# Two sums of squares by accumulating transfers, and another queue for y

## The reference

```python
# q, k, v, a_re, a_im: [4, 8, 768, 48]
mag = np.sqrt(a_re * a_re + a_im * a_im)
scale = np.minimum(mag, 0.999) / (mag + 1e-06)
a_re_n, a_im_n = a_re * scale, a_im * scale
for t in range(S):                       # complex decay of a 48 x 48 state per head
    new_re = ar * S_re - ai * S_im
    new_im = ar * S_im + ai * S_re
    S_re, S_im = new_re + k[t] (x) v[t], new_im
    y[:, :, t] = np.einsum('bhd,bhde->bhe', q[:, :, t], S_re)
# x = y as [3072, 384]
h = x @ w_in                             # 384 -> 2048
x = softplus(h) @ w_out                  # 2048 -> 384
out = ((x @ w1) * (x @ w2)) @ w3 @ w_out2
```

## Time and profile before

| | us |
|---|---|
| median of 3 runs | 1011.33 (1008.62 to 1012.21) |
| time of the profiled execution | 1010.65 |
| its span, first to last instruction | 1008.9 |
| PE busy | 912.0 (90%) |
| DVE busy | 607.4 (60%) |
| ACT busy | 426.8 (42%) |
| POOL busy | 70.4 (7%) |

### The profile page before, as it was taken

The page is one execution under the profiler, slowest core; times in us unless marked ns, Lnnn a source line. Parts: engine busy times, 40 slices in busy tenths (PEclk is TensorE's granted clock), DMA queues, the critical chain, the costliest instruction groups (busy, mean ns, idle before and its releaser), DMA issues.

```text
span 1008.9 us, 14507 instructions
## 1 busy us (share of the span) xinstructions
PE 912.0 (90%) x5442; PEld 828.5 (82%) x5442; DVE 607.4 (60%) x966; ACT 426.8 (42%) x618; POOL 70.4 (7%) x56
## 2 busy tenths in 40 slices
PE   0964839999999999999989999987999999999998
PEld 0533739988999888989889999987888888888887
DVE  5977978989989989989899723445121212121211
ACT  3152254673764664853854654667011111212011
POOL 0000000000000000000000000000222222222221
PEclk9985569999999999999999999999999999999999
DMA  9676074381470570560650630232101010101000
GB/s 338 227 201 176 20 205 110 106 196 55 137 207 13 152 192 10 169 176 13 196 145 12 174 78 12 72 124 79 32 1 63 1 63 0 62 0 63 1 32 32
DMA packets 98663, 99.52 MB, mean 99 GB/s; under 512 B 6944, under 2 KB 91936, under 8 KB 98592
## 3 DMA queue, kind: packets, MB, share of 16 engines
q1 hardware_dynamic: 98592, 98.59, 34.1%
HBM read 63.96 MB, written 29.88 MB: 93 GB/s over the span
## 4 chain that ended last, share of the span: by engine, by line
PE 47%; DVE 28%; DVEq 9%; ACT 8%; issue 4%; DMA 3%; ACTq 1%; SPq 0%
PE ps_p L1281 5%; PE ps_p L1282 5%; PE ps_p L1283 5%; DVE sp L1165 4%; DVEq L921 3%; PE ps L1469 3%; PE ps L1467 3%; PE ps L1468 3%; DVE g_l L1172 2%; DVE am L1119 2%; PE ps L1281 2%; PE ps L1283 2%; PE ps L1282 2%; PE ps_ay L1317 2%; DVE an L953 2%
## 5 line engine op out<-in xcount | busy, mean ns | idle before, releaser
L1281 PE MATMUL ps<-g_h,wo_h 128*128 128x384 f32 x384 | 133.5, 348 | 7.1 <-DVE g_l L1172 7.1
L629 POOL TENSOR_TENSOR abl<-ab,abh 128x512 fp32r<-128x512 f32 x48 | 69.5, 1447 | 931.7 <-DVE abh L1263 931.7
L1281 PE MATMUL ps_p<-x1h,win_h 128*128 128x384 f32 x336 | 117.3, 349 | 15.7 <-DVE sp L1165 15.3
L1283 PE MATMUL ps<-g_h,wo_l 128*128 128x384 f32 x384 | 129.4, 337 | 0.0
L1282 PE MATMUL ps<-g_l,wo_h 128*128 128x384 f32 x384 | 129.1, 336 | 0.0
L1283 PE MATMUL ps_p<-x1h,win_l 128*128 128x384 f32 x336 | 113.1, 337 | 0.0
L1282 PE MATMUL ps_p<-x1l,win_h 128*128 128x384 f32 x336 | 113.0, 336 | 0.0
L745 ACT ACTIVATE g_h<-sp 128x768 fp32r<-128x768 f32 (+1 forms) x71 | 55.5, 781 | 98.2 <-DVE sp L1165 98.2
L1317 PE MATMUL ps_ay<-stq,stk 96*128 96x128 f32 x384 | 57.5, 298 | 34.7 <-DMA vt<-in_v 13.3
L1254 DVE TENSOR_TENSOR ab<-ps_ay,bc 128x512 f32<-128x512 f32 x24 | 16.6, 693 | 117.0 <-ACT bc L892 117.0
L1317 PEld LDWEIGHTS ps_ay<-stq,stk 96*128 96x128 f32 x384 | 54.9, 211 | 35.9 <-issue 23.4
(11 more groups left out here) (147 smaller groups left out, 2053.4 us busy)
## 6 DMA issues: line engine op xcount, KB each, us to landing
qk_scr<-tt SPq DMA_DIRECT2D x16, 576.0 KB, 4.5
stq<-qk_scr SPq DMA_DIRECT2D x48, 192.0 KB, 4.8
qk_scr<-pp SPq DMA_DIRECT2D x16, 576.0 KB, 4.1
stk<-qk_scr SPq DMA_DIRECT2D x48, 192.0 KB, 4.6
an<-in_a_re SPq DMA_DIRECT2D x8, 576.0 KB, 4.1
an<-in_a_im SPq DMA_DIRECT2D x8, 576.0 KB, 5.2
qk<-in_q SPq DMA_DIRECT2D x8, 576.0 KB, 7.5
qk<-in_k SPq DMA_DIRECT2D x8, 576.0 KB, 8.7
```

The lines of the kernel that those rows point to most:

```text
L629: tensor_tensor(abl[:, m % AR, :], ab[:, m % 2, :], abh[:, m % AR, :].bitcast(F32), ALU.subtract).then_inc(ab_lo, 1)
L1281: mm(o, wh, xh, start=start, stop=False)
L1283: return mm(o, wl, xh, start=False, stop=stop)
```

## The change

Both sums of squares leave VectorE. GpSimd, once the squares are there, begins a transfer that reads the second half of `te` and adds it onto the first half, and ScalarE waits for 16 on the semaphore where it waited for 1. `prep_m2_` and `prep_p2_` become empty. `store_y` moves from SyncE to GpSimd, with the waits that stood before it. GpSimd's order is that in which the work falls due: in tile m's attention, the sum for p of tile m + 1 after block 3 and the sum for a of tile m + 2 after block 4. Nothing else is moved.

```diff
--- before.py
+++ after.py
@@ -409,13 +409,6 @@
                     eng.dma_start(stk[D * i:D * i + D, :, cs], qk_scr[2 + i].rearrange("(h d) t -> d h t", d=D)[:, :, cs])\
                         .then_inc(k_rd[c], 16)
 
-            def store_y(m, i):
-                c, hq = i // 2, i % 2
-                wait(y_ev, NG * m + i + 1)
-                for u, row, rows, pairs, p0, gs_ in Y_MOVES[hq]:
-                    eng.dma_start(x1raw[p0:p0 + rows, gs_, CT * c:CT * c + CT], ys[64 * u + row:64 * u + row + rows, i % 2, pairs, :])\
-                        .then_inc(y_wr[i], 16)
-
             def load_x1(n, m):
 
                 for c0, rows, p0, g in PLACES:
@@ -467,10 +460,6 @@
             wait(w34_ev, NM2)
             eng.dma_start(w34_scr.rearrange("c p n -> p c n"), w34s[:, :, :]).then_inc(w34_wr, 16)
             load_piece(7)
-
-            wait(raw_lo, 5)
-            for i in range(NG):
-                store_y(0, i)
             wait(prep_p, 4)
             load_a(2)
             store_q(1)
@@ -486,29 +475,17 @@
 
                 if not first:
                     store_x2(n - 1)
-                if att:
-
-                    if first:
-                        wait(x1_lo, 2)
-                    else:
-                        x2_landed(n - 1)
-                    for i in range(NG - 2):
-                        store_y(n + 1, i)
                 if prep:
                     wait(prep_p, 2 * n + 6)
                     if nxt:
                         load_a(n + 3)
                     store_q(n + 2)
-                if att:
-                    store_y(n + 1, NG - 2)
                 if prep:
 
                     wait(yz_mm, NG * n + NG + 4)
                     for c in range(2):
                         stack_q(n + 2, c)
                         load_v(n + 2, c)
-                if att:
-                    store_y(n + 1, NG - 1)
                 if prep:
                     store_k(n + 2)
                     for c in range(2):
@@ -629,6 +606,45 @@
                 tensor_tensor(abl[:, m % AR, :], ab[:, m % 2, :], abh[:, m % AR, :].bitcast(F32),
                               ALU.subtract).then_inc(ab_lo, 1)
 
+            def store_y(m, i):
+                c, hq = i // 2, i % 2
+                eng.wait_ge(y_ev, NG * m + i + 1)
+                for u, row, rows, pairs, p0, gs_ in Y_MOVES[hq]:
+                    eng.dma_start(x1raw[p0:p0 + rows, gs_, CT * c:CT * c + CT], ys[64 * u + row:64 * u + row + rows, i % 2, pairs, :])\
+                        .then_inc(y_wr[i], 16)
+
+
+            def sum_squares(m):
+                eng.wait_ge(prep_sq, m + 1)
+                eng.dma_start(te[:, 0, :], te[:, 1, :], accum_op=ALU.add).then_inc(prep_m2, 16)
+
+            def sum_psquares(m):
+                eng.wait_ge(prep_psq, m + 1)
+                eng.dma_start(te[:, 0, :], te[:, 1, :], accum_op=ALU.add).then_inc(prep_p2, 16)
+
+            sum_squares(0)
+            sum_psquares(0)
+            sum_squares(1)
+
+            eng.wait_ge(raw_lo, 5)
+            for i in range(NG):
+                store_y(0, i)
+            sum_psquares(1)
+            sum_squares(2)
+            for m in range(1, NT):
+
+                if m == 1:
+                    eng.wait_ge(x1_lo, 2)
+                else:
+                    for mo in range(G):
+                        eng.wait_ge(x2_wr[mo], 16 * m)
+                for i in range(NG):
+                    store_y(m, i)
+                    if m < NT - 1 and i == 3:
+                        sum_psquares(m + 1)
+                    if m < NT - 2 and i == 4:
+                        sum_squares(m + 2)
+
             with eng.Fori(0, NT2) as t:
                 for m in range(NM2):
                     ab_low(t, m)
@@ -659,7 +675,7 @@
                 last.then_inc(prep_sq, 1)
 
             def prep_log(m):
-                eng.wait_ge(prep_m2, m + 1)
+                eng.wait_ge(prep_m2, 16 * m + 16)
                 act(te[:, 1, :], te[:, 0, :], ACT.Ln)
 
             def prep_root(m):
@@ -688,7 +704,7 @@
                     prep_psquare(m, i)
 
             def prep_inverse(m):
-                eng.wait_ge(prep_p2, m + 1)
+                eng.wait_ge(prep_p2, 16 * m + 16)
                 act(te[:, 1, :], te[:, 0, :], ACT.Ln)
                 eng.drain()
                 act(stats[:, 5 * m + 2:5 * m + 5].unsqueeze(2), by_g(te[:, 0, :])[:, :, T - 1:T], ACT.Copy).then_inc(end_ev, 1)
@@ -924,9 +940,7 @@
                 eng.drain()
 
             def prep_m2_(m):
-                eng.wait_ge(prep_sq, m + 1)
-                ve.tensor_tensor(te[:, 0, :], te[:, 0, :], te[:, 1, :], ALU.add).then_inc(prep_m2, 1)
-                eng.drain()
+                pass
 
             def prep_newton(m):
 
@@ -1013,9 +1027,7 @@
                 ve.tensor_tensor(tt[:, :, :], qk[:, 0:1, :].to_broadcast([P, 2, GT]), pp[:, :, :], ALU.mult).then_inc(prep_q, 1)
 
             def prep_p2_(m):
-                eng.wait_ge(prep_psq, m + 1)
-                ve.tensor_tensor(te[:, 0, :], te[:, 0, :], te[:, 1, :], ALU.add).then_inc(prep_p2, 1)
-                eng.drain()
+                pass
 
             def prep_inv_newton(m):
 
```

## The result

The change makes the kernel slower: 1095.2 us, median of 4 runs (1093.3 to 1098.4), against 1011.8 of the kernel before; ratio 1.083, 95% interval 1.081 to 1.085. The profiled execution has a span of 1096.6 us, 87.7 more than before; it is the slowest of the four (1098.4), so its losses add up to some 4 us more than the medians'.

The account below looks back on a forecast made before the run. It put 47% of the span on TensorE and 28% on VectorE. Terms 31.2 + 22.0 + 19.4 + 5 = 77.6 us on 1010.65 gave 1088 us, own range 1065 to 1105, 8 in 10 between 1036 and 1140.

Parts of the forecast that it names:

- Two waits of ScalarE, passed on: Before both Ln ScalarE waits for the transfer; TensorE then idles 4 to 5 us twice in a slot.
- |p|^2, 5.2 us late: Slots 0 to 5: the |p|^2 transfer takes 7.0 us, making its Ln 5.2 us late, six times: 31.2 us.
- |a|^2, 4.4 us late: Slots 0 to 4: the |a|^2 transfer takes 6.0 us, making its Ln 4.4 us late, five times: 22.0 us.
- Start, 19.4: Before the slots, four late sums (7.6, 4.2, 4.1, 3.5 us) count in full; |a|^2 of tile 2 counts nothing: 19.4 us.
- Clock, 5: TensorE's lower clock after new stops costs 1 us in each of five slots: 5 us.
- y at nothing: y's 192 issues moving from SyncE to GpSimd count 0, with +4 us a slot as upper end.
- A: Rival: the addition lands like a plain copy, in 3.6 us; 24.6 us in all, 1035 us; chance 0.20.
- The estimate of 4.7 us: Transfer time for 1.18 MB by the skill's rule and straight line; the sum would be about 41 us, 1051 us.
- B: Rival: the transfer is slow, 10 us like the k load in a full queue; 125 us, 1136 us; chance 0.15.
- C: Rival: GpSimd's issues at 2 us each hold up the |a|^2 sum by 3.8 us; 19 us on top, 1107; chance 0.10.
- D: Rival: transfers land within 1.84 us (|p|^2) and 1.57 us (|a|^2); VectorE's 14.9 us come back, 996 us; chance 0.05.

Follow-up runs that it names:

- sums_alone: Kernel after, with y's moves back on SyncE, so only the two sums become GpSimd's accumulating transfers; 1094.2 us, ratio 1.082.
- hidden_p2: Kernel after, with |a|^2 summed on VectorE and the next step's softplus ahead of the |p|^2 Ln, other preparation later; 1049.7 us, ratio 1.037.
- m2_alone: Kernel after, with the sum of |p|^2 back on VectorE, so only |a|^2 is summed by a transfer; 1052.0 us, ratio 1.040.
- quiet_p2_alone: Kernel after, with |a|^2 summed on VectorE and SyncE's next a loads and q-product store held until the |p|^2 sum lands; 1057.6 us.
- y_alone: Kernel before, with only y's moves put on GpSimd and both sums still VectorE additions; 1013.7 us, ratio 1.0016.
- quiet: Kernel after, but in the slots SyncE begins the next a's loads and q-product store only once the |p|^2 sum has landed; 1095.7 us.
- sliver: Kernel after, but each transfer adds only 16 of 1152 columns (8 KB) and VectorE the other 1136 beside it; 1047.6 us, ratio 1.036.
- q_on_pool: Kernel before, with the product of q and the decays made by GpSimd instead of VectorE; 1023.2 us, ratio 1.012.
- copy: Kernel after, but VectorE adds |p|^2 and ScalarE's Ln also waits for GpSimd's plain copy of the same 576 KB; 1075.5 us, ratio 1.063.

## Why the prediction was right

The time (1088 forecast, 1095 measured) was right, and so was the mechanism in the main: ScalarE waits for transfers that land too late, and TensorE loses by it. The terms were less so; too small and too large ones partly cancel:

- **Two waits of ScalarE, passed on.** Shown: `sums_alone` has all of the loss, the releaser of both idle times is the transfer, `hidden_p2` takes away most of the |p|^2 wait and 20 us with it. Slot 6 didn't change, as said. The way from ScalarE to TensorE was another than I had it: not softplus and its sum come too late first, but the mask of the scores behind the inverse (6.24 us at 316.14), and when the up-projection is due at 319.32 its sum is ready. And TensorE doesn't stop twice for 4 to 5 us in a full slot, it stops once for 6.2 to 7.0 us (`m2_alone`, above, has what became of the second stop).
- **|p|^2, 5.2 us late.** Too small. I took 7.0 us from the end of the squares to the Ln, it is 8.5 to 9.1: 6.7 to 7.1 us late, with a wait of 6.8 to 7.2. The sharing was mis-sized: alone it would be 5.3 (`quiet_p2_alone`), so the traffic adds 3.2 or more us and not 1.5. Slot 5 lost 8.9 for my 5.2.
- **|a|^2, 4.4 us late.** Near: 5.4 to 6.2 us for my 6.0, waits of 3.2 to 3.9. Together a full slot lost 10.5 us where I had 10.6 with the clock. That this agrees so well is luck: |p|^2 was too small by nearly 2 us, |a|^2 too large by some 0.6, and the clock was sized otherwise than it came.
- **Start, 19.4.** Measured 24 (34.65 with slot 0, less its 10.5). Gaps of 10.3, 7.4, 5.3 and 8.6 us where the kernel before has 1.4, 2.8, 2.9 and 3.5 make 21, and the one sum that I counted at nothing, |a|^2 of tile 2, is 2.6 us later.
- **Clock, 5.** The lower level came as said, but costs TensorE more than the 1 us a slot that I took: in slots 1 to 4 it is busy for 2.9 to 3.7 us longer than before, in slot 5, where no |a|^2 wait follows, for 2.6 us of its 8.9 (and idle for 6.3). In full slots the loss is also about the sum of ScalarE's two waits (slot 2 lost 10.3 for 6.85 + 3.60). The two accounts meet because the slower work and the second wait lie in the same time; what a full slot would lose at the full clock, no run shows.
- **y at nothing.** Shown: +1.7 us (`y_alone`).
- **Rivals.** A, a transfer as quick as a copy: the plain copy itself, at this place, lands in 5.7 us and not 3.6. The estimate of 4.7 us that stood beside my sum is near the transfers with little beside them (4.9 for |a|^2, 5.1 in `quiet`), but the one for |p|^2 takes 8.4. B, 10 us: only the first transfer of all needs that (9.9). C, GpSimd's issues: 0.52 us each, under the 1.37 that I gave them, and none of a y move took over 0.61 in the kernel after, so nothing held GpSimd's issues up there. D, that the transfer could land under its cover, is excluded by `sliver`: with 8 KB it still needs 4.9 us at |p|^2 for 1.84 of cover and 2.1 at |a|^2 for 1.57.

## What to carry to other kernels

An addition of 1.35 us on an engine that is nearly always busy was still the cheap place, because its result was wanted within 2 us: before moving an operation to a transfer, read the time between the end of its input and the start of its consumer, and what stands behind the consumer in an in-order queue. A transfer of this kind has a floor that a smaller size doesn't remove (2.1 us for 8 KB here), and other traffic raises it; keeping that traffic away pays only if it doesn't meet the next waiting transfer. Relief of a busy engine can't be counted where that engine then waits for another one: VectorE's 20 us shortened no slot of the kernel after. And a stop of TensorE can cost more than its length, by the slower clock behind it (2.6 us in slot 5).

## What the runs showed of the hardware

- An accumulating transfer begun by GpSimd costs its queue 0.92 to 0.96 us to issue, the plain copy of the same size 0.58, a y move 0.52.
- GpSimd doesn't issue transfers ahead without end. In the kernel after, four of the six moves of block 4 are issued at once, the last two only when the sum has landed, 4.59 us later; in `quiet`, where the sum lands sooner, they stand only 1.45 us. ScalarE had no wait for them. What limits it isn't shown. GpSimd's timeline in the kernel after:

```profile
301.65 0.97 POOL L623 DMA_DIRECT2D te<-te  x1 [6.13 <-ACT te L698]
303.49 2.04 POOL L613 DMA_DIRECT2D x1raw<-ys  x4 [0.87 <-ACT ys L737]
310.12 0.99 POOL L613 DMA_DIRECT2D x1raw<-ys  x2 [4.59 <-issue]
```

- Two elementwise instructions with both inputs in the on-chip memory, one on GpSimd and one on VectorE, hardly ran beside each other: in `q_on_pool` VectorE's took 2.91 us for 1.35, GpSimd's its usual 5.15. VectorE's two before it, which read one of their inputs from TensorE's results (the mask from ps_ay, the sum from ps_p), took their usual 0.69 and 0.96 beside the same GpSimd instruction. The Trainium skill (SBUF — State Buffer, "Who interferes with whom") states that VectorE's second input and GpSimd's reads share an interface; the trace agrees.
- The last slot, which has no attention, took between 48.6 us (`copy`) and 53.4 us (kernel after) for 51.95 before, though its work was the same in all. The granted clock goes with it in part: 1.00 in `copy`, 0.97 before, 0.94 in the kernel after, with TensorE busy for 46.8, 48.3 and 49.6 us. But `m2_alone` took 50.5 us at 1.00; the rest is open.
